# Attention values summed before they are scaled, by inverses that TensorE transposes, with tiles handled two at a time

## The reference

```
q, k, v: (2, 8, 768, 64)                     # batch, heads, positions, head dim
s = q @ k.T / 8 + bias[head]                 # ALiBi-like; only 8 global columns and the last 96 positions are kept
a = exp(s - max(s));  a = a / (sum(a) + 1e-9)
x = (a @ v) -> (1536, 512)
x = silu-MLP(x):      h = x @ w_in (512x2048);  (h * sigmoid(h)) @ w_out (2048x512)
x = hard-swish-MLP(x) with its own weights:     (h * clip(h + 3, 0, 6) / 6) @ w_out
```

## Time and profile before

| | |
|---|---|
| median of 3 runs | 600.92 us (600.9 to 602.3) |
| the profiled execution | 600.91 us, span 599.2 us |
| TensorE busy | 590.4 us, 99% |
| VectorE, ScalarE, GpSimd busy | 373.2, 341.8, 284.8 us |
| TensorE clock granted | 1.00 of full speed throughout (2.4 GHz) |
| attention part | from the first scores at about 5.6 us to the last values at 99.9 us |

### The profile page before, as it was taken

The page is one execution under the profiler, slowest core; times in us unless marked ns, Lnnn a source line. Parts: engine busy times, 40 slices in busy tenths (PEclk is TensorE's granted clock), DMA queues, the critical chain, the costliest instruction groups (busy, mean ns, idle before and its releaser), DMA issues.

```text
span 599.2 us, 9614 instructions
## 1 busy us (share of the span) xinstructions
PE 590.4 (99%) x3429; PEld 514.0 (86%) x3429; DVE 373.2 (62%) x696; ACT 341.8 (57%) x659; POOL 284.8 (48%) x353
## 2 busy tenths in 40 slices
PE   7999999999999999999999999999999999999998
PEld 4665568999999999999999998888888988889896
DVE  7778876867655668547555775575557675554331
ACT  6999885544455657534544674454547565555441
POOL 4888995569533334369333144394333343331110
PEclk9999999999999999999999999999999999999999
DMA  8435330121221122222222122122221252121002
GB/s 349 170 134 189 108 120 25 60 105 59 91 70 59 65 71 71 71 72 71 71 72 71 36 78 71 64 70 71 71 70 36 71 188 74 56 71 36 1 1 105
DMA packets 14595, 50.05 MB, mean 84 GB/s; under 512 B 1618, under 2 KB 1874, under 8 KB 14546
## 3 DMA queue, kind: packets, MB, share of 16 engines
q1 hardware_dynamic: 14258, 48.63, 23.8%
q10 hardware_dynamic: 288, 0.79, 0.4%
HBM read 46.27 MB, written 3.15 MB: 82 GB/s over the span
## 4 chain that ended last, share of the span: by engine, by line
PE 88%; POOL 5%; DVE 3%; ACT 1%; issue 1%; DMA 0%; DVEq 0%; ACTq 0%
PE ps L967 38%; PE ps L1045 22%; PE ps L1036 14%; PE ps L1037 7%; POOL probs L304 3%; PE ps L939 2%; PE ps L914 2%; PE ps L924 2%; POOL rsume L296 1%; ACT probs L695 1%; DVE g_lo L622 1%; DVE g_f L501 0%; DVE wi_lo L476 0%; POOL x_t L341 0%; POOL x_t L336 0%
## 5 line engine op out<-in xcount | busy, mean ns | idle before, releaser
L349 POOL TENSOR_TENSOR wo_lo<-wo_raw,wo_hi 128x1024 fp32r<-128x1024 f32 x32 | 77.0, 2406 | 261.4 <-ACT wo_hi L762 255.0
L967 PE MATMUL ps<-x_hi,wi_hi 128*128 128x384 f32 x448 | 151.1, 337 | 0.5 <-DVE g_f L501 0.3
L967 PE MATMUL ps<-x_hi,wi_lo 128*128 128x384 f32 x448 | 150.0, 335 | 0.0
L967 PE MATMUL ps<-x_lo,wi_hi 128*128 128x384 f32 x448 | 150.0, 335 | 0.0
L491 DVE TENSOR_TENSOR c_sb<-ps,p_c 128x384 f32<-128x384 f32 x64 | 35.7, 557 | 159.7 <-PE ps L967 159.5
L742 ACT ACTIVATE p_c<-ps 128x384 f32<-128x384 f32 x64 | 31.5, 492 | 128.1 <-PE ps L967 127.8
L967 PEld LDWEIGHTS ps<-x_hi,wi_hi 128*128 128x128 f32 x448 | 84.1, 188 | 4.4 <-ACT u_c L742 1.0
L967 PEld LDWEIGHTS ps<-x_hi,wi_lo 128*128 128x128 f32 x448 | 84.1, 188 | 0.7
L967 PEld LDWEIGHTS ps<-x_lo,wi_hi 128*128 128x128 f32 x448 | 84.1, 188 | 0.0
L1045 PE MATMUL ps<-wo_hi,g_lo 128*128 128x512 f32 (+1 forms) x194 | 76.3, 393 | 0.0
L1045 PE MATMUL ps<-wo_lo,g_hi 128*128 128x512 f32 (+1 forms) x194 | 76.3, 393 | 0.0
(11 more groups left out here) (94 smaller groups left out, 1092.9 us busy)
## 6 DMA issues: line engine op xcount, KB each, us to landing
wi_raw<-in_w_in SPq DMA_DIRECT2D x32, 512.0 KB, 3.4
wo_raw<-in_w_out SPq DMA_DIRECT2D x32, 512.0 KB, 3.4
v_raw<-in_v SPq DMA_DIRECT2D x8, 704.0 KB, 4.1
k_raw<-in_kT SPq DMA_DIRECT2D x8, 464.0 KB, 5.0
out_y<-y_out SPq DMA_DIRECT2D x11, 256.0 KB, 4.3
q_raw<-in_qT SPq DMA_DIRECT2D x6, 384.0 KB, 5.5
q_raw<-in_qT ACTq DMA_DIRECT2D x2, 384.0 KB, 4.1
out_y<-y_out SPq DMA_DIRECT2D x2, 128.0 KB, 1.9
```

Of the source, the lines that this page charges most:

```text
L349: nc.gpsimd.tensor_tensor(wo_lo[:, s % 2, :], wo_raw[:, s % 2, :], wo_hi[:, s % 2, :], ALU.subtract).then_inc(wo_lo_ok, 1)
L967: mm = nc.tensor.matmul(p_bank(bank), w[:, s % 2, at], x[:, b, k, :], start=fresh and k == 0 and i == 0, stop=k == 1 and i == 2, skip_grou ...
```

## The change

1. Probabilities are no longer normalised. `turn_probs(u)` transposes the plain exponentials and waits for `exps` alone. The two `norm` instructions per unit go.
2. The inverse is applied to the sums of values. GpSimd spreads four inverses over 64 columns each (`spread(r)`, 128x256), TensorE transposes that (`turn_inverses(r)`, two transposes), ScalarE copies it to SBUF (`copy_inverses(r)`, 128x256), and VectorE multiplies the values in PSUM by it on the way to `x_raw` (`x_scaled(r)`, 128x256). `x_copy` goes.
3. Everything runs in **rounds** of two units: round r holds units 2r and 2r + 1 (`NR` = 24 rounds). TensorE's round r: scores of both its units, transposes of units 2r - 4 and 2r - 3, inverses of round r - 3, values of round r - 4. `total` and `inverse` handle both units in one instruction.
4. `copy_t` of even units is on ScalarE, of odd units on VectorE; `probsT` has six buffers, `negs` three, `probs` six instead of seven.
5. GpSimd makes the first operands: `w_high` and `w_low` of steps 0 and 1, `x_high` and `x_low` of four of the seven x operands, and the score biases. The second `wo_high` moves into step 1 of the MLP loop. The products of step 0 are interleaved with the last three rounds in another way.

```diff
-            def norm(u):
-                pool.wait_ge(inv_ok, u + 1)
...
+            def spread(r):
+
+                pool.wait_ge(inv_ok, r + 1)
+                at_least(pool, turned_ok, r - 1)
+                at = slice(2 * r % DEEP, 2 * r % DEEP + 2)
+                nc.gpsimd.tensor_scalar(rinv64[:, r % 2, :].rearrange("p (n d) -> p n d", d=D),
+                                        rinv[:, at, :].rearrange("p u h -> p (u h)").unsqueeze(2).broadcast_to([P, 4, D]),
+                                        1.0, 1.0, ALU.mult, ALU.mult).then_inc(spread_ok, 1)
...
+            def x_scaled(r):
+
+                dve.wait_ge(pv_done, r + 1)
+                nc.vector.tensor_tensor(x_pair(r), o_bank(r)[:, 0:2 * P], inverses[:, r % 2, :], ALU.mult).then_inc(x_ok, 1)
...
+                for r in range(NR):
+                    u = 2 * r
+                    if r >= 4:
+                        x_scaled(r - 4)
                     if u % NT == 0 and 0 < u < 4 * NT:
-                        dve.wait_ge(bias_ok, 2 * (u // NT) + 1)
...
+                    for k in (u, u + 1):
+                        negated(k, 0)
+                        if k == 0:
+                            dve.wait_ge(bias0_ok, 1)
+                        negated(k, 1)
+                    if r >= 2:
+                        inverse(r - 2)
+                    if r in (1, 2):
+                        copy_t(2 * r - 1)
+                    if r >= 4:
+                        copy_t(2 * r - 3)
...
                 for u in range(NU):
-                    if turned(u) is not None and turned(u) % 3 == 0:
-                        copy_t(turned(u))
                     exps(u)
...
+                    if u in SOON_COPY:
+                        copy_t(SOON_COPY[u])
+                    if u >= 10 and u % 2 == 0:
+                        copy_t(u - 4)
+                    if u >= 6 and u % 2 == 0:
+                        copy_inverses(u // 2 - 3)
...
             def turn_probs(u):
-                pe.wait_ge(norm_done, 2 * (u + 1))
+                pe.wait_ge(exp_done, 2 * (u + 1))
                 if u >= 2:
                     pe.wait_ge(*copied(u - 2))
...
+                for r in range(3, NR):
+                    scores(r)
+                    turn_probs(2 * r - 4)
+                    turn_probs(2 * r - 3)
+                    turn_inverses(r - 3)
+                    if r >= 4:
+                        values(r - 4)
```

More of the change, by code:

```diff
@@ L123, in build @@
                 probs = sb("probs", [P, DEEP, 2, 256], F32, banded)
-                probsT = sb("probsT", [P, 2, 4, P], F32, banded)
+                probsT = sb("probsT", [P, 6, 4, P], F32, banded)
+                inverses = sb("inverses", [P, 2, 2 * P], F32, banded)
                 negmax = sb("negmax", [P, DEEP, 2], F32, banded)
@@ L291, in _, with total @@
             io = dict(allow_small_or_imprecise_dtypes=True)
[L293 to L297, removed]
-            def norm(u):
-                pool.wait_ge(inv_ok, u + 1)
[L302 to L305, removed]
+            def total(r):
+                pool.wait_ge(exp_done, 4 * (r + 1))
+                at_least(pool, inv_ok, r - 2)
+                at = slice(2 * r % DEEP, 2 * r % DEEP + 2)
+                nc.gpsimd.tensor_scalar(rsume[:, at, :], rsum[:, at, :], EPS, 1.0, ALU.add, ALU.mult).then_inc(sum_ok, 1)
@@ L367, in banded @@
             def banded():
[L368 to L377, removed]
+                pool.wait_ge(base_ok, 1)
+                for r in range(NR):
+                    if r < 3:
+                        bias(2 * r + 2)
+                        bias(2 * r + 3)
+                    total(r)
+                    work = W_WORK.get(r, ()) + X_WORK.get(r, ())
+                    for i, (kind, which, part) in enumerate(work):
+                        if i == 1:
+                            spread(r - 1)
+                        if r in W_WORK:
+                            if kind == "s":
+                                w_sum(which, part)
+                            elif kind == "h":
+                                w_high(which, part)
+                            else:
+                                w_low(which, part)
+                        else:
+                            if kind == "s":
+                                x_sum(0, which, part)
+                            elif kind == "h":
+                                x_high(which)
+                            else:
+                                x_low(which)
+                    if r and len(work) < 2:
+                        spread(r - 1)
+                spread(NR - 1)
                 for half in range(2):
@@ L527, in banded @@
                 base()
-                for u in range(NU):
+                for r in range(NR):
+                    u = 2 * r
+                    if r >= 4:
+                        x_scaled(r - 4)
                     if u % NT == 0 and 0 < u < 4 * NT:
-                        dve.wait_ge(bias_ok, 2 * (u // NT) + 1)
[L531 to L539, removed]
-                        copy_t(turned(u))
[L541 to L548, removed]
+                        dve.wait_ge(bias_ok, 2 * (u // NT))
+                    for k in (u, u + 1):
[9 more added lines that the diff above has]
+                        copy_t(2 * r - 3)
+                inverse(NR - 2)
+                copy_t(NU - 3)
+                inverse(NR - 1)
+                x_scaled(NR - 4)
+                x_low(0, B22)
+                c_sum(0, 0, 1, p1_c, P2)
+                copy_t(NU - 1)
+                x_scaled(NR - 3)
                 x_low(0, T3)
-                c_sum(0, 0, 1, p1_c, P2)
-                copy_t(NU - 2)
+                x_scaled(NR - 2)
                 x_low(0, T4)
-                copy_t(NU - 1)
+                c_sum(0, 1, 0, p5_c, P7)
+                silu(0, 0)
+                c_sum(0, 2, 1, u2_c, P3)
+                for n in range(1, 4):
+                    silu(0, n)
+                x_scaled(NR - 1)
             def general():
@@ L822, in general @@
                 keep(0, p1_c, 0, P1)
-                for s in range(2):
-                    wo_high(s)
+                wo_high(0)
                 keep(0, u2_c, 0, P6)
```

234 lines of the change are left out of this document (128 added, 106 removed).

## The result

The changed kernel takes 622.64 us (median of 4 runs, 622.55 to 622.75), the kernel before 601.61 us beside it on the same chip (4 runs, 600.9 to 602.68). The ratio is 1.0348, with a 95% interval of 1.0329 to 1.0368: slower by 3.5%, 21.0 us. The prediction said 619, with a range of 612 to 625.

A forecast was written before the change was run, and what follows sets the result against it. It took a ring of waits through VectorE, ScalarE and TensorE to bound attention after the change: first x_scaled 16.75, round 23 at 102.5, last values 118.0 us against 99.93, so 18.1 us later, 619 us, range 612 to 625.

The forecast's parts named there:

- The mechanism: In attention, TensorE's transposes wait for ScalarE's probsT copy, VectorE's x_scaled for TensorE's values; TensorE stands about 1.5 us per round.
- the ring: Attention loop x_scaled, negated, exponentials, ScalarE's copy, transposes, values, back to x_scaled: 4.85 us per full round.
- the first-tile term: First-tile units shorten negated, exponentials, ScalarE's copy, transposes and values: 1.00 us off per three rounds, 13.55 us in all.
- hand-over 0.04: Passing from VectorE's accumulator to ScalarE's exponentials, and from ScalarE's copy to TensorE, was put at 0.04 us each.
- The start: Attention's first rounds: first negated at 6.83 us as before, first values 16.65, first x_scaled at 16.75 us.
- The tail: From round 23's start on VectorE at 102.5 us to the last values at 118.0, TensorE's final 13.2 us running unheld.
- The sum: Attention's last values end at 118.0 us against 99.93, later by 18.1 us, giving 619 us.
- At nothing: Costs put at zero: GpSimd's biases and operand splits (longest 2.1 us), the second wo_high, later loads; MLP length unchanged.
- TensorE running through (1): Rival: no cyclic wait holds in attention, TensorE never stands, 8 us earlier, 593 us; 6 in 100.
- GpSimd late (2): Rival: eight long GpSimd splits stretch to 4 us, costing 0.8 us each, 625 us; 8 in 100.
- A shorter ring (3): Rival: the ring holds but is 0.2 to 0.5 us less per round over 18 rounds, 610 to 615 us; 14 in 100.
- the expected gain: TensorE's attention work falls from 10.42 to 9.64 us per three rounds, 0.78 us less, 6.2 us in 24 rounds.

The follow-up runs named there:

- e1_x_late: Changed kernel with x_scaled(r - 4) moved from the head of VectorE's round to its end, behind copy_t; 596.74 us.
- e4_late_noinv: e1_x_late without spread, turn_inverses and copy_inverses, VectorE copying the values unscaled, so attention is not divided by its sums; 593.7 us.
- e5_late_qk: e1_x_late with the loads of the next head pair's k and q issued ahead of the wait for v's buffer; 593.74 us.
- e7_spread_slow: Changed kernel with GpSimd's spread as a slower two-input addition of the inverses to themselves, the total doubled to make up for it; 622.84 us.
- e2_copy_first: Changed kernel with ScalarE's copy_t and copy_inverses ahead of the exponentials of unit 2r instead of behind them; 617.96 us.
- e3_late_split: e1_x_late with TensorE taking scores and transposes per unit again, two more changes of kind per round, same matmuls; 602.06 us.
- e6_x_mid: Changed kernel with x_scaled(r - 4) between the negated of the round's first and second unit; 605.9 us.

## Why the prediction was right, point by point

- **The mechanism.** Right in each link: L986 waits for L774 in 19 places, L582 for L1010 in 19, and e1_x_late gives the whole loss back and more by cutting the link. The wait per round was put at "about 1.5 us", and is 1.4 (26.5 in 19).
- **The size of the ring.** Predicted 4.85 us for a full round and 1.00 us off in three. The trace has 4.39, 4.73 and 4.74 for three rounds (54.90, 59.29, 64.02, 68.76), and from its steps a full round is 0.34 + 0.54 + 1.00 + 0.68 + 2.38 = 4.94, so 0.96 off in three: the first-tile term was close. The step that was mis-sized is the hand-over, "hand-over 0.04" twice. The accumulator ends at 60.05 and ScalarE starts at 60.17, so 0.12; ScalarE's copy ends at 61.74 and the weight load starts at 61.85, so 0.11. Together they are 0.15 more than the sum had; `x_scaled` (0.34 for 0.36) and the copy (0.57 for 0.60) took 0.05 less. The 0.04 came from another pair, VectorE's copy to TensorE's values. Rounds 5 to 22 took 83.4 us and not 81.3:

```profile
22.44 0.42 DVE L582 TENSOR_TENSOR x_raw<-ps,inverses 128x256 f32<-128x256 f32 x1 [2.06 <-PE ps L1010]
...
105.88 0.42 DVE L582 TENSOR_TENSOR x_raw<-ps,inverses 128x256 f32<-128x256 f32 x1 [2.27 <-PE ps L1010]
```

- **The start.** "First `x_scaled` at 16.75" was 17.91, the largest single miss (1.16 us), because "first `negated` at 6.83 as now" did not hold: it starts at 7.80. The first scores in the chain of the changed kernel (eight matmul records, those of two units), and VectorE's row behind them:

```profile
5.55 2.10 PE ps L976 x8
```

```profile
7.80 0.29 DVE L564 CUSTOM_DVE_ANT_0 negs<-ps,m_bias 128x128 f32<-128x128 f32 x1 [1.03 <-PE ps L976]
```

The same eight records also started at 5.55 before and took 1.14 us. In e4_late_noinv alone of the rearranged kernels they ran at the old pace (5.71 to 6.87), and there the first `negated` stands at 7.01:

```profile
7.01 0.29 DVE L565 CUSTOM_DVE_ANT_0 negs<-ps,m_bias 128x128 f32<-128x128 f32 x1 [0.24 <-PE ps L977]
```

Its k landed 0.16 us later (5.71 for 5.55), and that is nearly all by which 7.01 exceeds 6.83. So the slow scores, 0.96 us longer, make up practically the whole 0.97. They count in full because unit 0 now waits for both units' scores, which share one signal. At the slow pace unit 0's own half would have ended near 6.6 (an estimate, 5.55 and half of 2.10), early enough; a separate signal for it wasn't tried, since the scores of both units share a PSUM bank.

The slow pace is not new with the scores. In every kernel here, the one before too, TensorE starts with it; what differs is how far it reaches. Weight loads of eight 128x128 transposes in the kernel before take 1.57 us at the start, where the changed kernel's take 0.86 at 66.38. In e5_late_qk all sixteen records of the first two rounds are slow, 3.78 us where later ones take 1.06 for eight:

```profile
1.42 1.57 PEld L898 LDWEIGHTS ps<-ident 128*128 128x128 f32 x8 [1.42 <-POOL ident L289]
```

```profile
5.69 3.78 PE ps L977 x16
```

That is near half pace. TensorE at the lower of its two clock levels would look like this, but the profile has a granted clock of 1.00 in all these stretches, so the cause stays open.

- **The tail.** 15.5 us from the start of round 23 to the end of the last values (102.5 to 118.0), measured 15.7 (105.88 to 121.6).
- **The sum.** The last values end at 121.6 and not at 118.0: 1.2 from the start, 2.1 from the ring, 0.3 elsewhere. From 99.93 that is the span's 21.7 us.
- **At nothing.** Right: the MLP is as long as before, `w_low` took 2086 ns where 2.1 us was estimated, `spread` 403 ns where 0.49 us was.
- **The rivals.** TensorE running through (1) is what e5_late_qk does, at the price given, but not the changed kernel. GpSimd late (2) is refuted by the waits, where GpSimd releases TensorE once, for 0.7 us, and by e7_spread_slow, where 0.2 us more on GpSimd in each round cost nothing. A shorter ring (3) is what e2_copy_first makes by hand: 617.96 us, above the 610 to 615 that the rival was given. Its 4.7 us less than the changed kernel are 0.26 for each of 18 rounds, within the 0.2 to 0.5 named; the times were low because they were counted down from 619. The granted clock stayed at 1.00 (2.4 GHz) though TensorE was busy 70% only; the one place where its pace was low is the start, above.
- **Where the expected gain went.** The prediction put it at 0.78 us per three rounds, 6.2 us, and it was there: e5_late_qk ends 7.1 us below the kernel before. The rearrangement saves three changes of mode per round. Two of them are worth 5.3 us over the kernel (e3_late_split); the third, at the values, no run took back. The turned inverses cost 3 to 6 us of it (e4_late_noinv), and the 2.5 us of waits for normalised probabilities went too, which was not tested by itself. The ring hid the whole gain, and late loads hid 3 us more (e5_late_qk).

## What to carry to other kernels

When work moves to another engine, don't add up the engines' loads alone: write down for each engine the order of one round, and follow from each waiting instruction who is queued behind it and who waits for that. Where the walk comes back to its start, the sum of that ring is the least that a round can take, however small the loads are. An instruction that only drains a result, like `x_scaled` here, belongs at the end of its engine's round, behind everything that feeds the next one. And once a stall is gone, look at the queue that issues the loads: a load that needed no buffer stood behind one that did, and came late as soon as rounds were shorter.

## What the runs showed of the hardware

- A hand-over between engines has no single price. In the changed kernel's ring VectorE to ScalarE took 0.12 us and ScalarE's copy to TensorE's weight load 0.11. From VectorE's copy to TensorE it was 0.04 us ahead of the values in the kernel before, and in e6_x_mid 0.11 to the weight load and 0.14 to the transpose, though TensorE had stood idle for about as long (0.25 and 0.32 us). From TensorE's last value to VectorE it was 0.02, though VectorE had been idle for 2.3 us. So idle time alone does not set it; what does was not isolated. TensorE's rows, before and in e6_x_mid, where VectorE's copy ends at 51.23 us:

```profile
88.94 0.66 PE L939 MATMUL ps<-probsT,v_raw 128*64 128x128 f32 x8 [0.25 <-DVE probsT L523]
```

```profile
51.34 0.42 PEld L986 LDWEIGHTS ps<-ident,probs 128*128 128x128 f32 x4 [0.53 <-ACT probs L763]
51.37 0.63 PE L986 MATMUL ps<-ident,probs 128*128 128x128 f32 x4 [0.32 <-DVE probsT L577]
```

- The first eight score records took 2.10 us in place of 1.14, at a granted clock of 1.00 in both, in the changed kernel; the slow pace is there from TensorE's first transposes on in every kernel, and ends before the first scores in two of nine profiles (the kernel before and e4_late_noinv).
- A change between score matmuls (64x128), transposes (128x128) and value matmuls (128x64) costs TensorE 0.17 us, also where nothing is waited for: 2.44 against 2.09 us for the same 16 records in four groups or in two. A new group of the same mode, the inverses' transposes behind those of the probabilities, showed no such cost.
